# An attention, feed-forward and mixture-of-experts kernel: a shorter look-ahead and another order around the start of the dense loop, a later bookkeeping step on GpSimd, and two SBUF spacers taken out

## The reference, cut to what matters

```
# 1: attention with a decaying state, B=4, H=8, S=768, D=48
for t in range(S):
    cur   = u * k[t] (x) v[t]
    y[t]  = r[t] @ (state + cur)
    state = w * state + k[t] (x) v[t]
# 2: dense layer on x = y as [3072, 384]:  silu(x @ w_in) @ w_out, inner width 2048
# 3: top-1 mixture of 8 experts, inner width 1024
logits = x @ w_gate + modality_bias[modality_id]
e_idx  = argmax(logits);  gate_w = softmax(logits)[e_idx]
out[mask] = gate_w[mask] * (relu(x[mask] @ w1[e]) @ w2[e])
```

## Time and profile before

| | us |
|---|---|
| median of 3 runs (789.14 to 790.64) | 790.36 |
| the profiled execution | 790.64 |
| its span in the profile | 789.1 |
| PE busy | 743.5 |
| DVE busy | 500.2 |
| ACT busy | 420.8 |
| POOL busy | 229.2 |

### The profile page before, as it was taken

One profiled execution on the slowest core, in us unless ns is written; L12 is line 12 of the kernel. 1 busy time (PEld: TensorE's weight loads), 2 busy tenths in 40 slices (PEclk: granted clock), 3 DMA queues, 4 the chain that ended last, 5 costly groups with the idle time before them and its releaser, 6 DMA issues. The chain is left out here.

```text
span 789.1 us, 24974 instructions
## 1 busy us (share of the span) xinstructions
PE 743.5 (94%) x9894; PEld 723.3 (92%) x9894; DVE 500.2 (63%) x1349; ACT 420.8 (53%) x1076; POOL 229.2 (29%) x350
## 2 busy tenths in 40 slices
PE   3599999999999999999999999997998999999994
PEld 3498899999999999999999999996898999999994
DVE  7889765856585657655666657226865666556662
ACT  4776555555454646455555554435554665566652
POOL 4531222332124222422233212102414333334330
PEclk9599999999999999999999999997999999999997
DMA  8951222222122222222212210413575765665561
GB/s 315 382 181 39 95 76 96 75 66 89 55 96 75 95 77 96 75 95 74 69 69 95 76 59 3 149 53 120 193 194 193 266 233 199 237 247 218 213 226 56
DMA packets 24159, 104.94 MB, mean 133 GB/s; under 512 B 4411, under 2 KB 9800, under 8 KB 20482
## 3 DMA queue, kind: packets, MB, share of 16 engines
q1 hardware_dynamic: 19362, 93.34, 33.3%
q0 software_dynamic: 4704, 10.29, 3.8%
HBM read 93.90 MB, written 10.11 MB: 132 GB/s over the span
## 5 line engine op out<-in xcount | busy, mean ns | idle before, releaser
L636 ACT ACTIVATE g<-ps_h 128x256 f32<-128x256 f32 x192 | 73.5, 383 | 204.7 <-PE ps_h L1027 174.3
L1025 PE MATMUL ps_h<-x_hi,wi_hi 128*128 128x256 f32 x576 | 164.5, 286 | 5.2 <-DVE x_lo L808 5.1
L1026 PE MATMUL ps_h<-x_lo,wi_hi 128*128 128x256 f32 x576 | 162.1, 281 | 0.0
L1027 PE MATMUL ps_h<-x_hi,wi_lo 128*128 128x256 f32 x576 | 161.8, 281 | 0.0
L1042 PE MATMUL ps_o<-wo_hi,g_hi 128*128 128x392 f32 x384 | 135.4, 352 | 2.6 <-DVE g_lo L841 1.5
L1043 PE MATMUL ps_o<-wo_lo,g_hi 128*128 128x392 f32 x384 | 130.5, 340 | 0.0
L1044 PE MATMUL ps_o<-wo_hi,g_lo 128*128 128x392 f32 x384 | 130.5, 340 | 0.0
L841 DVE TENSOR_TENSOR g_lo<-g,g_hi 128x256 fp32r<-128x256 f32 x192 | 81.8, 428 | 70.3 <-ACT g_hi L629 68.4
L507 POOL TENSOR_TENSOR store<-store,up_half 128x256 f32<-128x256 f32 x44 | 34.3, 780 | 312.5 <-PE ps_y L1012 310.4
L1025 PEld LDWEIGHTS ps_h<-x_hi,wi_hi 128*128 128x128 f32 x576 | 109.7, 190 | 7.2 <-DVE x_lo L808 5.3
L1027 PEld LDWEIGHTS ps_h<-x_hi,wi_lo 128*128 128x128 f32 x576 | 109.9, 191 | 0.0
(11 more groups left out here) (199 smaller groups left out, 1524.5 us busy)
## 6 DMA issues: line engine op xcount, KB each, us to landing
store<-in_w SPq DMA_DIRECT2D x28, 1536.0 KB, 9.1
store<-in_quads SPq DMA_DIRECT2D x48, 704.0 KB, 4.7
x_rows<-rows SPq DMA_DIRECT2D x12, 384.0 KB, 3.0
woT_raw<-in_woT SPq DMA_DIRECT2D x4, 768.0 KB, 10.4
wi_raw<-in_wi SPq DMA_DIRECT2D x4, 768.0 KB, 10.3
wo_raw<-in_wo SPq DMA_DIRECT2D x4, 768.0 KB, 11.4
store<-x_rows,entries POOLq DMA_INDIRECT x26
out_rows<-y,entries_out POOLq DMA_INDIRECT x26
```

Of the source, the lines that this page charges most:

```text
L636: S.activation(g[:, F % 2, :], ps_h[F % 2][:, 0:ETOK], ACT.Silu).then_inc(g_made, 1)
L1025: T.matmul(out, hi, x_hi[:, t % 2, c, :], start=(c == 0), stop=False)
L1026: T.matmul(out, hi, x_lo[:, t % 2, c, :], start=False, stop=False)
L1027: last = T.matmul(out, lo, x_hi[:, t % 2, c, :], start=False, stop=(c == KC - 1))
```

## The change

Five edits; the arithmetic is the same.

1. `x_place` is gone, and `warm` (4 floats) stands between `x_lo` and `g`. `x_hi` and `x_lo` so lie 1344 bytes lower in each partition, `g`, `g_hi`, `g_lo` and `rows` 1312 bytes lower. In the experts block `xe_place` is gone, and `xe_hi`, `xe_lo`, `h_hi`, `h_lo` and `y` lie 992 bytes lower. (Offsets of the starts: `x_hi` from 173248 to 171904, `g_hi` from 187584 to 186272, `xe_hi` from 108064 to 107072, `h_hi` from 114208 to 113216.)
2. On ACT `first_states` moves from ahead of the loop to slot 0, behind `g_high(0)`.
3. On ACT and DVE the look-ahead of `wi_high` and `wi_low` is 4 chunks, not 6.
4. On DVE `x_low(3)` moves behind `scale(4)` and `sum_bonus(4)`.
5. On POOL `results_landed(1)` and `shift_entries(1)` move behind the wait for the lists and `load_entries(table, 3)`.

```diff
-        sb("x_place", [P, 336])
         x_hi = sb("x_hi", [P, 2, KC, ETOK], F32R)
         x_lo = sb("x_lo", [P, 2, KC, ETOK], F32R)
+        warm = sb("warm", [P, 4])
         g = sb("g", [P, 2, ETOK])
...
-        warm = sb("warm", [P, 4])
...
             x_high(3)
-            first_states()
             wi_high(3)
-            wi_high(4)
-            wi_high(5)
             for F in range(SLOTS):
...
                 g_high(F)
+                if F == 0:
+                    first_states()
...
-                if F < FCH - 6:
-                    wi_high(F + 6)
+                if F < FCH - 4:
+                    wi_high(F + 4)
...
             wi_low(2)
-            x_low(3)
             scale(4)
             sum_bonus(4)
+            x_low(3)
             wi_low(3)
-            wi_low(4)
-            wi_low(5)
...
-                if F < FCH - 6:
-                    wi_low(F + 6)
+                if F < FCH - 4:
+                    wi_low(F + 4)
...
-        sb("xe_place", [P, 248])
...
-            results_landed(1)
-            shift_entries(1)
             tiles = tiles_with_tokens(pool)
             pool.wait_ge(listed, 16 * TB)
             load_entries(table, 3)
+            results_landed(1)
+            shift_entries(1)
```

## The result

| | before | after |
|---|---|---|
| median of 4 runs each, us | 790.35 (789.14 to 790.64) | 800.55 (799.39 to 802.55) |
| profiled execution, us | 790.64 | 802.33 |
| its span, us | 789.1 | 800.7 |

A forecast was written before the change was run, and what follows sets the result against it. DVE was taken to set the end of tile 0, and PE everything behind it up to the experts. 790.64 + 2.3 (front) + 0 (POOL) + 0 (placement) = 792.9, median forecast 792.7 us, range 788.8 to 796.8.

The forecast's parts named there:

- The placement: Matmuls of dense and expert tiles: new operand offsets taken to change nothing, 0, with bounds from two spacings seen before.
- rival 4: Matmuls of dense and expert tiles: the placement is worse, up to 4.8 us more, 797.5 us; chance 0.09.
- all at 0.1175: Slow bound for up matmuls, every one at 0.1175 us: 1.7 us more in the dense layer, 0.7 in the experts.
- x_low(3) behind scale(4): DVE before the loop: the moved scale(4) and sum_bonus(4) start PE 1.55 us later, at 35.25.
- if POOL hinders both: High end for PE's later start, with scale pieces and x_low(3) both slowed beside POOL: 2.55 us.
- first_states in slot 0: ACT in slots 0 and 1: scale_b(5) ready at 44.6, scores(5) waits 0.3 us more, PE 1.85 us late.
- Look-ahead 4: DVE in tile 0: two more chunks in its full stretch, 2 x 0.46 = 0.92 us more.
- POOL: Experts' third tile: the later shift delays the scaling of results by 1.7 us, but costs PE 0.
- The cover: Experts' third tile: PE's 1.75 us gather wait absorbs the late scaling; without it, up to 1.7 us lost.
- Rival 1: Tile 0: the front does not bind, the delay shrinks below 1.5 us, 791.2 us; chance 0.13.
- Rival 2: Front: the full clock comes later, PE works 8.7 us longer at half clock, 4.95 late, 795.3 us; chance 0.15.
- Rival 3: Matmuls 128x256: placement gives the short spacing, 789.1 us for experts alone, 783.1 with dense tiles; chance 0.21.

The follow-up runs named there:

- a1: The changed kernel with both spacers and warm back in their old places, the four moves of work kept: 795.34 us, ratio 1.0069 to the kernel before.
- e1: The kernel before with the placement edits alone (x_place and xe_place out, warm between x_lo and g): 796.29 us, ratio 1.0074.
- q4: The kernel before with x_hi, x_lo, xe_hi and xe_lo at offset 0 modulo 256, all else where it was: 795.5 us, one execution.
- e2: The kernel before with only x_low(3) moved behind scale(4) and sum_bonus(4): 793.14 us, ratio 1.0030.
- u1: The kernel before with scale(4) alone ahead of x_low(3), sum_bonus(4) staying behind it: 792.25 us, ratio 1.0014.
- s1: The kernel before with first_states alone moved from ahead of the loop into slot 0: 791.20 us, ratio 1.0015.
- s2: The kernel before with only the look-ahead of wi_high and wi_low cut from 6 chunks to 4: 791.38 us, ratio 1.0019.
- e4: The kernel before with only results_landed(1) and shift_entries(1) moved behind load_entries(table, 3): 790.95 us, ratio 1.0006.
- e3: The kernel before with first_states in slot 0 and look-ahead 4 together: 793.92 us, ratio 1.0043.
- q2: The kernel before with g_hi at 160 and h_hi at 64 modulo 256, x_hi and xe_hi keeping theirs: 788.2 us, one execution.
- b1: The kernel before with g_hi at 160 modulo 256, the other operands keeping their offsets: 789.37 us, ratio 0.9988.
- u2: The kernel before with g_hi at 160 modulo 256 and POOL's products of quad 5 held until x_low(3) is done: 789.22 us, ratio 0.9981.
- q3: The kernel before with x_hi, x_lo at 64 and xe_hi, xe_lo at 192 modulo 256, all else where it was: 791.9 us, one execution.

## Why the prediction was wrong

**The placement** was the step that failed most. The prediction took it at 0, and gave rival 4, a worse placement, a chance of 0.09 and at most +4.8 us. It is +5.2 to +5.3 by the medians (a1, e1). The bounds were made of the two spacings that the earlier trace rows show, 0.113 and 0.1175 us, with "all at 0.1175" as the worst. But 0.1175 is the worst of that one placement: others have a mean of 118.5 and up to 120.2 ns. By the spacings of the table the 1728 dense up matmuls pay 1728 x 2.0 ns = 3.5 us, the 936 of the experts 0.7, and the 624 down matmuls of the experts 624 x 3.1 = 1.9: 6.1 us, a little above what is measured. The down steps were allowed 2.4 in all, a little more than they cost; the dense up steps cost twice their bound of 1.7. The sentence that two alignments gave nearly the same mean was true, and no evidence: 192 and 32 are the two best offsets of eight. Nor did it follow from two spacings behind the same `x_hi` that the address does not matter: the spacing varies within a tile, and the address moves its mean.

The Trainium skill, page "SBUF — State Buffer", section "Who interferes with whom", says that PE waits on nobody for SBUF. The prediction doubted it for the right reason and then still centred on its answer; the spacing of the up matmuls moved by 2 to 3% with nothing but addresses (q4, 119.1 for 116.5 and 120.2 for 117.2). Whether PE waits for another engine then, or its own reads take longer, no run shows.

**x_low(3) behind scale(4)** was mis-sized: +1.55 forecast, 2.2 by the two profiles and 2.1 to 2.45 by e2. The high bound of 2.55, "if POOL hinders both", was near the true case. In the changed kernel the moved work takes 2.9 us where it took 1.55, beside POOL, and the pieces of `x_lo` give back only 0.35 us (1.95 for 2.30). The prediction held that POOL's two products would end at 33.4 in either order, which they nearly did (33.1); it did not ask what the moved `sum_bonus(4)` sets free. It is a step for which POOL's next product waits, and that product now runs beside the pieces of `x_lo`. u1 shows it: without the early release they take 1.31 us, with it 1.9.

**first_states in slot 0** was right up to `scores(5)`. With the measured start instead of the forecast one (0.67 later) the chain gives 45.3, and `scores(5)` ran at 45.21. But PE came to it at 44.0, 0.3 us earlier than the prediction had it although its start was 0.7 later; the clock rose at 42.3 as before, so that less of PE's work fell into the half clock. And one link was missing: "behind slot 1 ACT is as late as PE was at the start". ACT is as late as `bonus(5)`, for which `set_diagonal(5)` waits. That is where the 1.1 us by which s1's stretch begins late comes in.

**Look-ahead 4**: the mechanism was right (two more chunks on DVE, and DVE decides the end of the tile), the price was not. 2 x 0.46 was taken from rows with POOL quiet; s2 paid about 1.8. That DVE's idle time takes up 0.2 us, as the prediction has it, no profile shows.

So for the front the forecast was +2.3 and the moves are +5.1: 0.6 to 0.9 for DVE beside POOL at the start, 0.9 for the dearer chunks (1.1 with the 0.2 taken off), 1.1 for the link that was missing. These are readings of single profiles, and by the scatter of tile 0 their sum is good to about 1 us. The side of the forecast was no luck, since the moves alone are slower by 5.1 us; its size was short in the front as well: with the old placement (a1, 795.3) it would have been 2.6 us short, but inside its range, and the placement took it out.

**POOL** was right: 0, measured 1.0006 (0.9996 to 1.0017). The cover was not quite the one named. In the changed kernel PE's wait at the gather turned into one of 2.43 us for `h_lo` behind the scaling; in e4 PE loses 0.78 us at `h_lo` and still waits 1.46 us at the gather, and the fourth tile gives the loss back (17.39 us for 19.09). Why the fourth tile does so was not looked for.

**The rivals.** Rival 1 (the front does not bind) fell in e2 and e3. Rival 2 (the clock comes back later) did not happen in the front: 42.3 for 42.4 us. Rival 3 (faster placement) is out for this placement, though q2 and b1 point to a better one, worth about 1 us. Rival 4 was the one that came, on top of a front that cost twice its forecast, and at the end of its bounds or over it. Of the marks named in advance, the wait of about 6 us ahead of `wi_low(4)` (5.73), the order of the rows and the rise of the clock were met; the first up step (35.92 for 35.25), the end of tile 0 (91.2 for 88) and the spacings were not. "If the steady dense tiles or the expert tiles change their length" was named as a sign of being wrong, and it is the one that came.

## What to carry to other kernels

Spacers that nobody reads may carry the address of a matmul operand: before one is taken out, compare the spacing of the matmuls in two or three other placements, since the spread of one placement did not bound that of the others here (0.1175 us at most in the one, means of up to 0.1202 in the others). When an instruction is moved ahead, ask also what its semaphore sets free and what that then runs beside. Price added work on an engine at what it costs beside its neighbour's bursts, and follow a late chain one link past the wait that you were looking for.

## What the runs showed of the hardware

- The mean distance of neighbouring float32r matmuls 128x256 is 115.9 to 120.2 ns, depending mostly on the place of the moving operand in SBUF (its offset modulo 256 bytes in this table); that of matmuls 128x384 is 173.4 to 176.7 ns, following the place of the stationary one. Over this kernel that is some 7 us between a good and a bad placement (q2 is 1.2 under before, q4 6.1 above it, one execution each).
- A subtraction on DVE with both inputs in SBUF takes 0.96 us beside a product on POOL and 0.55 alone (128x384, s2), and the three pieces of `x_lo` take 1.9 to 2.3 (e2, before) against 1.3 (u1, u2). The Trainium skill, page "SBUF — State Buffer", section "Who interferes with whom", has that the two contend; the rows agree.
- The granted clock went from 0.5 (1.2 GHz) to 1.0 (2.4 GHz) at 42.3 us in the changed kernel and at 42.4 in the one before, with up steps that began 2.2 us apart, and at 39.5 in u2, whose up steps began at 31.97. The rise does not follow the start: with up steps from 33.1 to 33.7 us it came anywhere from 39.7 (q3) to 42.9 (e3). The windows of u2 on both sides of it, with the columns of the earlier trace rows:

```profile
32.00:39.40 7.40, 6.56 (x103) 5.78 (x104) 7.40 (x15) 4.95 (x13) 4.44 (x6) 0.50 1.04 413
39.60:60.00 20.40, 18.56 (x352) 17.64 (x351) 18.03 (x40) 15.89 (x46) 6.53 (x8) 1.00 0.44 160
```

What sets the time of the rise was not looked for.
